# Attention, a gated MLP and a routed MLP in one kernel: one PSUM bank per head for the scores, weights split on GpSimd, another order of first loads

## The reference

```
# attention, q, k, v of (4, 8, 576, 64); heads 0 to 3 local, 4 to 7 strided
scores = q @ k^T / 8
mask_local   = (rel >= 0) & (rel < 32)
mask_strided = (rel >= 0) & (pos_q % 32 == pos_k % 32)
attn = softmax(where(mask, scores, -1e9)); x = attn @ v        # then (2304, 512)
# MLP 1, w_in (512, 1024), w_out (1024, 512)
h = x @ w_in; s = h * softmax(h); x = layernorm(s) * g_ln @ w_out
# MLP 2, eight experts, one chosen per token by argmax(x @ w_gate + bias)
out = gate * (relu(x @ w1[e]) @ w2[e])
```

## Time and profile before

| | us |
|---|---|
| median of 3 runs | 623.78 (623.58 to 623.84) |
| profiled execution | 621.45 |
| its span | 619.7 |
| TensorE busy | 594.2 (96%) |
| VectorE busy | 309.5 (50%) |
| ScalarE busy | 234.0 (38%) |
| GpSimd busy | 146.2 (24%) |

### The profile page before, as it was taken

How to read it: one execution, slowest core, us unless ns; L and a number is a source line. 1 busy time by engine, 2 the same in 40 slices (tenths; PEclk the granted TensorE clock), 3 DMA queues, 4 the chain that set the end, 5 groups by cost and what they waited for, 6 DMA issues and landing times.

```text
span 619.7 us, 11298 instructions
## 1 busy us (share of the span) xinstructions
PE 594.2 (96%) x3655; PEld 491.2 (79%) x3656; DVE 309.5 (50%) x735; ACT 234.0 (38%) x728; POOL 146.2 (24%) x151
## 2 busy tenths in 40 slices
PE   5999999999999999999999999979999999999995
PEld 4677777767888888888888888878998987788894
DVE  5999999866665766566655513642211200021210
ACT  3888888833333333434343421211221211111210
POOL 5555555540010001422342101000011021101001
PEclk9999999999999999999999999999999999999999
DMA  8867666200000070000000000009400026100000
GB/s 183 182 169 171 163 160 162 80 0 19 17 31 21 21 285 19 34 17 17 21 30 17 18 18 32 16 24 403 165 34 17 32 93 250 33 16 31 15 16 34
DMA packets 69035, 47.47 MB, mean 77 GB/s; under 512 B 54840, under 2 KB 56856, under 8 KB 69008
## 3 DMA queue, kind: packets, MB, share of 16 engines
q1 hardware_dynamic: 66928, 41.08, 22.9%
q0 software_dynamic: 2080, 6.03, 2.7%
HBM read 37.66 MB, written 10.22 MB: 77 GB/s over the span
## 4 chain that ended last, share of the span: by engine, by line
PE 77%; issue 9%; POOL 6%; DVE 3%; SPq 2%; DMA 1%; ACT 1%; POOLq 0%; DVEq 0%; ACTq 0%
PE bank L573 16%; PE bank L986 16%; PE pair L971 16%; PE pair L573 15%; POOL work L545 4%; PE pair L1612 3%; PE pair L1622 3%; PE pair L1079 2%; POOL w_lo L552 2%; PE bank L1099 1%; SPq L422 1%; DMA arena<-in_k 1%; PE pair L1111 1%; PE pair L694 1%; PE bank L705 1%
## 5 line engine op out<-in xcount | busy, mean ns | idle before, releaser
L971 PE MATMUL pair<-x_hi,lead_hi 128*128 128x256 f32 x288 | 83.1, 288 | 1.3 <-DVE lead_h L1031 1.3
L971 PE MATMUL pair<-x_lo,lead_hi 128*128 128x256 f32 x288 | 82.1, 285 | 0.0
L971 PE MATMUL pair<-x_hi,lead_lo 128*128 128x256 f32 x288 | 82.1, 285 | 0.0
L765 ACT ACTIVATE work<-pair,neg_max 96x128 f32<-96x128 f32 (+2 forms) x176 | 61.6, 368 | 18.4 <-PE bank L705 14.6
L1520 POOL TENSOR_TENSOR rstd<-ln_small 128x1 f32 (+1 forms) x18 | 26.4, 1467 | 171.4 <-DVE ln_small L640 171.4
L1042 POOL DMA_INDIRECT out<-work,lead_sidx x18 | 17.9, 993 | 204.3 <-ACT work L1026 173.1
L573 PE MATMUL pair<-w_hi,x_hi 128*128 128x512 f32 x144 | 58.4, 406 | 0.2 <-ACT arena L754 0.2
L971 PEld LDWEIGHTS pair<-x_hi,lead_hi 128*128 128x128 f32 x288 | 56.0, 194 | 2.0 <-DVE lead_h L1031 1.5
L545 POOL TENSOR_TENSOR work<-work,row_inv 96x512 f32<-96x512 f32 (+3 forms) x48 | 44.8, 932 | 54.2 <-DVE row_inv L853 54.2
L573 PE MATMUL bank<-w_hi,lnT_hi 128*128 128x512 f32 x144 | 56.4, 391 | 1.1 <-DVE lnT_lo L1273 1.1
L573 PE MATMUL pair<-w_hi,x_lo 128*128 128x512 f32 x144 | 56.5, 392 | 0.0
(11 more groups left out here) (217 smaller groups left out, 1210.3 us busy)
## 6 DMA issues: line engine op xcount, KB each, us to landing
entry<-in_moe_w SPq DMA_DIRECT2D x12, 1024.0 KB, 7.8
arena<-in_q SPq DMA_DIRECT2D x32, 144.0 KB, 2.8
arena<-in_k SPq DMA_DIRECT2D x32, 144.0 KB, 3.2
x_dram<-work SPq DMA_DIRECT2D x18, 256.0 KB, 2.0
arena<-in_moe_w SPq DMA_DIRECT2D x8, 512.0 KB, 7.7
arena<-in_v SPq DMA_DIRECT2D x16, 144.0 KB, 2.6
work<-in_v SPq DMA_DIRECT2D x16, 135.0 KB
arena<-in_moe_w_in SPq DMA_DIRECT2D x8, 256.0 KB, 3.1
```

Source lines behind the costliest of these rows:

```text
L765: ins = act.activation(probs[g % 2][0:rows, cols], score_ps[g % 2][0:rows, cols], ACT.Exp, bias=neg_max[g % 2][0:rows, n:n + 1], accum_out ...
L971: ins = pe.matmul(lead_h_ps[n % 2][:, jj * BLK:(jj + 1) * BLK], a[:, w], b[:, x], start=(passes == 1), stop=(passes == 3 * KC))
```

## The change

- `score_ps` of a group becomes a pair of banks, one per head. k is no longer block-diagonal: each head's scores come from a matmul of its own over its 64 partitions. The mask is written by two matmuls, one per bank. The turned probabilities and the values get one bank each, so each of them waits for the copy of the group before. The blocks of a group are ordered by head, then tile.
- `take_k` copies both heads at once. The memsets of `k_T` shrink to the 32 padding columns.
- The cast of the weights moves from ScalarE to GpSimd, into `rest_w`, and the splitting moves one step later: block i is split in step i+1, after groups 1 and 4; block 7 after the last step.
- On ScalarE, `take_o` comes ahead of `exps` in a slot.
- SyncE loads strided v of step 0 and the weights of block 0 after the q and k of step 1; `load_w(i)` is in step i.

```diff
-        k_T = [take(2 * (S + STRIDE)), take(2 * ST * SR)]
+        k_T = [take(S + STRIDE), take(ST * SR)]
...
-        score_ps = [pair0[:, 0:HALF], pair0[:, HALF:2 * HALF]]
+        score_ps = [pair0, pair1]
...
-        pT_ps = [bank[0], bank[1]]
-        o_ps = [pair1[:, 0:HALF], pair1[:, HALF:2 * HALF]]
+        pT_ps, o_ps = bank[0], bank[1]
...
+        def score_cols(g, hh, n=0, count=1):
+
+            keys = rows_keys(g)[1]
+            return score_ps[g % 2][0:rows_keys(g)[0], hh * HALF + n * keys:hh * HALF + (n + count) * keys]
...
-                if not (static(i) and i == NI - 1):
-                    sp.wait_ge(w_rounded, 2 * i + 1)
-                    load_w(i + 1)
+                if static(i) and i == 0:
+                    load_v(0, 1)
+                else:
+                    sp.wait_ge(w_rounded, 2 * i - 1)
+                load_w(i)
...
             load_v(0, 0)
-            load_v(0, 1)
-            load_w(0)
             step(0)
...
             def rest_w(i, m):
 
+                if m == 0:
+                    pool.wait_ge(ld_w, 32 * (i + 1))
+                cols = bass.ds(i * HALF + m * KC * FF, HALF)
+                pool.tensor_copy(w_hi[:, cols], w_raw[:, cols]).then_inc(w_rounded, 1)
                 pool.wait_ge(w_rounded, 2 * i + m + 1)
-                cols = bass.ds(i * HALF + m * KC * FF, HALF)
                 pool.tensor_tensor(w_lo[:, cols], w_raw[:, cols], w_hi[:, cols].bitcast(F32), ALU.subtract).then_inc(split_w, 1)
 
             def step(i):
                 for g in range(NG):
                     normalise(i, g)
-                    if g == 2:
-                        rest_w(i, 0)
-                    if g == 5:
-                        rest_w(i, 1)
+                    if g in (1, 4) and not (static(i) and i == 0):
+                        rest_w(i - 1, g // 4)
 
             steps(pool, step, False)
+            rest_w(NI - 1, 0)
+            rest_w(NI - 1, 1)
...
-                full = score_ps[g % 2][0:rows, 0:2 * len(tiles) * keys]
-                pe.matmul(full, ident_bf[0:rows, 0:rows], mask_of(g), start=True, stop=False)
+                for hh in range(2):
+                    pe.matmul(score_cols(g, hh, 0, len(tiles)), ident_bf[0:rows, 0:rows], mask_of(g), start=True, stop=False)
                 for n, t in enumerate(tiles):
-                    ins = pe.matmul(score_ps[g % 2][0:rows, n * 2 * keys:(n + 1) * 2 * keys],
-                                    q_cols(local, t), k_cols(local, t), start=False, stop=(t == tiles[-1]))
+                    for hh in range(2):
+                        part = slice(hh * D, (hh + 1) * D)
+                        ins = pe.matmul(score_cols(g, hh, n), q_cols(local, t)[part], k_cols(local, t)[part],
+                                        start=False, stop=(t == tiles[-1]))
...
-                wait(pe, p_out, c - 1)
+                wait(pe, p_out, c)
...
-                wait(pe, o_out, c - 1)
+                wait(pe, o_out, c)
...
                 for g in range(NG):
+                    if lagged(i, g, 3):
+                        take_o(*lagged(i, g, 3))
                     if not (static(i) and i == NI):
                         exps(i, g)
                     if next_third(i, g):
                         take_q(*next_third(i, g))
-                    if lagged(i, g, 3):
-                        take_o(*lagged(i, g, 3))
...
-                    if g in (1, 3) and not (static(i) and i == NI):
-                        round_w(i, g // 2)
...
-            dve.memset(k_T[0], 0.0)
-            dve.memset(k_T[1], 0.0).then_inc(zeroed, 1)
+            dve.memset(k_T[0][:, 0:STRIDE], 0.0).then_inc(zeroed, 1)
...
-                heads = k_T[kind].rearrange("p (h n) -> p h n", h=2)
-                for hh in range(2):
-                    part = slice(hh * D, (hh + 1) * D)
-                    for dst, src in in_order(heads[part, hh, k_pad[kind]:], banks_of(n)[1][part], kind, m):
-                        ins = dve.tensor_copy(dst, src)
+                for dst, src in in_order(k_T[kind][:, k_pad[kind]:], banks_of(n)[1], kind, m):
+                    ins = dve.tensor_copy(dst, src)
```

More of the change, by code:

```diff
@@ L346, in k_cols @@
         def k_cols(local, t):
-            kt = k_T[0 if local else 1].rearrange("p (h n) -> p h n", h=2)
+            kt = k_T[0 if local else 1]
             if local:
-                return kt[:, :, t * JR:t * JR + P]
-            return kt[:, :, t * SR:t * SR + NA * RES[t]]
+                return kt[:, t * JR:t * JR + P]
+            return kt[:, t * SR:t * SR + NA * RES[t]]
+        def score_cols(g, hh, n=0, count=1):
+            keys = rows_keys(g)[1]
+            return score_ps[g % 2][0:rows_keys(g)[0], hh * HALF + n * keys:hh * HALF + (n + count) * keys]
         def in_order(cols, ps, kind, m):
@@ L371, in mask_of @@
             rows, keys = rows_keys(g)
-            return m[0:rows, :].rearrange("p (n c) -> p n c", n=4)[:, 0:2 * len(tiles), 0:keys]
+            return m[0:rows, :].rearrange("p (n c) -> p n c", n=4)[:, 0:2 * len(tiles):2, 0:keys]
         def steps(eng, body, lag):
@@ L702, in turn_probs @@
                 pe.wait_ge(normed, c + 1)
-                wait(pe, p_out, c - 1)
+                wait(pe, p_out, c)
                 for n in range(2 * len(tiles)):
-                    ins = pe.transpose(pT_ps[g % 2][0:keys, n * rows:(n + 1) * rows],
+                    ins = pe.transpose(pT_ps[0:keys, n * rows:(n + 1) * rows],
                                        probs[g % 2][0:rows, n * keys:(n + 1) * keys], ident[0:rows, 0:rows])
@@ L717, in values @@
                 pe.wait_ge(p_out, c + 1)
-                wait(pe, o_out, c - 1)
+                wait(pe, o_out, c)
                 for n, t in enumerate(tiles):
                     for hh in range(2):
-                        at_ = (2 * n + hh) * rows
-                        ins = pe.matmul(o_ps[g % 2][hh * D:(hh + 1) * D, n * rows:(n + 1) * rows],
+                        at_ = (hh * len(tiles) + n) * rows
+                        ins = pe.matmul(o_ps[hh * D:(hh + 1) * D, n * rows:(n + 1) * rows],
                                         v_tile(local, t, hh), probs_T[g % 2][0:keys, at_:at_ + rows],
@@ L762, in exps @@
                 wait(act, p_turned, c - 1)
[L763 to L767, removed]
+                for hh in range(2):
+                    for n in range(len(tiles)):
+                        at_ = hh * len(tiles) + n
+                        ins = act.activation(probs[g % 2][0:rows, at_ * keys:(at_ + 1) * keys], score_cols(g, hh, n),
+                                             ACT.Exp, bias=neg_max[g % 2][0:rows, at_:at_ + 1],
+                                             accum_out=row_sum[g % 2][0:rows, at_:at_ + 1])
                 ins.then_inc(exped, 1)
@@ L775, in take_o @@
                 nt = len(tiles)
-                src = o_ps[g % 2][:, 0:nt * rows]
+                src = o_ps[:, 0:nt * rows]
                 if local:
@@ L839, in maxima @@
                 dve.wait_ge(scored, c + 1)
-                dve.tensor_reduce(neg_max[g % 2][0:rows, 0:n],
-                                  score_ps[g % 2][0:rows, 0:n * keys].rearrange("p (n c) -> p n c", n=n),
+                heads = score_ps[g % 2][0:rows, :].rearrange("p (h m) -> p h m", h=2)[:, :, 0:n // 2 * keys]
+                dve.tensor_reduce(neg_max[g % 2][0:rows, 0:n].rearrange("p (h n) -> p h n", h=2),
+                                  heads.rearrange("p h (n c) -> p h n c", c=keys),
                                   AX.X, ALU.max, negate=True).then_inc(maxed, 1)
@@ L861, in take_p @@
                 dve.tensor_copy(probs_T[g % 2][0:keys, 0:2 * len(tiles) * rows],
-                                pT_ps[g % 2][0:keys, 0:2 * len(tiles) * rows]).then_inc(p_out, 1)
+                                pT_ps[0:keys, 0:2 * len(tiles) * rows]).then_inc(p_out, 1)
             def step(i):
```

## The result

The changed kernel takes 629.69 us (median of 627.15, 628.58, 629.69, 631.51 and 636.78) against 623.58 us before (median of five, 620.99 to 623.84): a ratio of 1.0102, 95% interval 1.0071 to 1.0134. The kernel is slower by 1%; I had forecast 621 and a gain.

The account below looks back on a forecast made before the run. VectorE and ScalarE nearly full, a chain over two slots was taken to set the attention loop; afterwards GpSimd's pieces. Start -1.8, loop -6 x 0.6, end +2.45 sum to -2.95 us: 620.8, rounded to 621, range 616.5 to 627.5.

Parts of the forecast that it names:

- Start: Start of attention: earlier q/k loads and paired scores bring step 1's scores to 23.4 instead of 25.20, saving 1.8 us.
- Loop: Attention loop, steps 1 to 6: period 13.8 us, 0.6 less than now.
- Pairs: Scores on TensorE: two heads' row halves run together, four pairs taking 0.43 us, not 0.85; 0.6 to the values.
- cast: GpSimd's weight cast in the loop: taken as 0.65 us, by the select, from a span of 0.53 to 1.16.
- piece: GpSimd's work for one weight block: cast 0.65, semaphore wait 0.15, subtract 1.27, together 2.0 us against 1.27.
- the wait in slot 4: Attention loop: TensorE waits for normalise in slot 4, at a period near 13.8 us.
- The term that was short: Loop, exps of group 1 to exps of group 4, 6.8 us: exps to its semaphore 1.54, inverse 0.54 before normalise.
- End: Last step and end: TensorE waits 3.7 us for the last weight split ahead of tile 0's second half; 2.45 us lost.
- the rival on the clock: End of attention: the wait drops TensorE's clock to 1.2 GHz, costing 2 us, giving 623, no change; chance 0.18.
- serial row halves: Scores: row halves don't overlap, TensorE binds, period 14.8 us, kernel 628.6; chance 0.12.
- the dear cast: GpSimd's cast costs more: from 0.86 us on the change loses, at 1.16 it gives 628; chance 0.15.
- the period of 13.1: Loop: GpSimd's work hides better and the two-slot chain binds, -7.7 in the loop, 616.7 us; chance 0.2.

Follow-up runs that it names:

- the weights part: Kernel before with only the new weight splitting (cast on GpSimd, one step late) and new load order: 632.34 us, ratio 1.0137.
- after_warm: Changed kernel plus nine extra identity matmuls of 512 columns ahead of the first transposes: 627.45 us, ratio 1.0082.
- scores_only: The change without its weight and load part (casts on ScalarE, splitting and loads as before): 622.56 us, ratio 0.9982.
- scores_pad_warm: Change without its weight and load part, plus step 0's products issued again over 128 partitions and nine identity matmuls ahead of the first transposes: 619.22 us, ratio 0.9942.
- own_step_pad: Changed kernel with weights split in their own step, loads as before, step 0's products issued again over 128 partitions: 624.51 us, ratio 1.0031.
- own_step: Changed kernel with each weight block split in its own step (cast still on GpSimd) and loads as before: 624.77 us, ratio 1.0021.

## Why the prediction was wrong

- **Start: the step that failed.** "Laid out slot by slot ... the scores of step 1 start at 23.4". I priced slots 0 and 1 at half rate and the slots behind them at the loop's durations, as before had them. With light scores the half rate stayed to 31 us: 29.04, 5.64 off. The load order was right in sign; with the weights part it gave 1.23.
- **Loop: right in mechanism, its term too large.** Period 14.10 against 13.8. Pairs (0.61 us to the values against 0.6), cast (0.61 against 0.65), piece (65.63 to 67.68, 2.05 against 2.0) and the wait in slot 4 stand as laid out. The term that was short is the first: from exps of group 1 (62.20) to its normalise (64.65) it is 2.45 us, not 2.08: the EPS add queues behind the next group's maximum (63.59, 0.69) on VectorE. That is 0.37, and what VectorE and ScalarE lost in work does not shorten it. The rest of the miss is step 1, which began at half rate: 29.04 to 44.04 is 15.00, 1.2 more than a period of 13.8.
- **End: right in its wait, wrong in what follows.** Wait 3.60 against 3.7, counted from exps of group 4 the split ended at 7.68 against 7.5 (the last cast took 1.15 beside VectorE's `x_lo` subtract, 130.90 to 132.05, not 0.61). Then I took 4.1 us for the way to the maximum (before: 3.93); mostly at half rate it was 6.72. The last step and end cost 6.40 instead of 2.45. A smaller term of that was too short ahead of the wait: from exps of group 0 to exps of group 4 of the last step I had 9.0, and it took 10.09 (116.08 to 126.17), as it had before (10.31, 113.28 to 123.59), with the first half of tile 0's matmuls laid between. This was the rival on the clock, which I priced at 2 (it is 2.78) and gave 0.18 as if it were a matter of chance; all four profiles with the wait unfilled show it, and the earlier trace rows already showed half rate behind standing still.
- **The other rivals** are refuted: serial row halves and the dear cast by the rows of 0.61, the period of 13.1 by 14.10.
- **No term at all** stood for MLP 1 beyond the attention: +1.59, a low stretch at 150 to 154, on the first matmuls behind tile 0's layernorm. The change does not explain it. From the maximum of tile 0 to the first matmul on `slot_col` the fourteen profiles show two lengths: 273.7 to 273.8 us in eight (among them before and after_warm, which has the wait at the end) and 275.2 to 275.4 in six, each with a low stretch at that same place (among them scores_only and scores_pad_warm, which have no wait). Before and after fell on different sides.
- The luck was bad in that term, and nothing hangs on it: without it the ledger still stands 8.2 us above before.
- I had one rival on the clock, and it stood at the end only. What I did not ask is what lighter work does to an engine whose rate had not risen yet. The Trainium skill (TensorE: Matmul & The Clock Gate, Part 1) has the gate follow how busy the engine has been; here TensorE had records all the time from 14 to 20 us and ran at half rate, so idle gaps alone did not tell.

## What to carry to other kernels

Work taken off TensorE near the start, or a wait put before dense work, has to be priced at both clock levels: look up in the trace until when records run at half rate, and ask what the change makes of the work that ended it. A transfer of work to an engine with idle time moves the last piece as well: follow that piece to the instruction that waits for it behind the loop, before counting what a period wins. And where a chain over two slots binds, an engine's smaller sum of work shows only if it shortens the queue in front of the chain's own instruction.

## What was unexpected on the hardware

- Extra work made a kernel faster: the products of step 0 issued twice, once over 128 rows, took the median from 622.56 to 620.76 us and the maximum of tile 0 from 133.25 to 129.07. Full-row and half-row scores differ by 5.12 us in the start of step 1 (25.32, 30.44), though at full rate the half-row form is the shorter by a third (0.61 against 0.95).
- Half-row matmuls of two heads do run in pairs: eight records of 128 columns in 0.61 us.
- A 128 x 512 cast from f32 to fp32r on GpSimd took 0.61 us, and 1.15 beside VectorE's subtract of two SBUF operands; in turn the EPS add took 1.12 us (at 123.02) beside GpSimd's subtract, and 0.15 alone.
- The same kernel differs from one execution to the next by more than most edits here gain. The scores part alone took 618.69 to 625.11 us, and 619.75 to 621.73 once step 0 is dense; but own_step_pad, just as dense there, took 620.89 to 630.09 and own_step 620.94 to 625.83, so the light scores are not shown to be the reason.
- A stretch of low clock that costs about 1.5 us came or stayed away in one and the same place of MLP 1, six times in fourteen profiles, whatever the kernel.
